# Rotary products of attention moved from VectorE to GpSimd, in a fused attention and two-layer kernel

## The reference, cut to what matters

```python
def _attn_ref(q, k, v):                       # (4, 8, 576, 64) each
    ...
    def rotate(x):
        x1, x2 = (x[..., :half], x[..., half:])
        return np.concatenate([x1 * cos - x2 * sin, x1 * sin + x2 * cos], axis=-1)
    q_rot, k_rot = (rotate(q), rotate(k))
    scores = scale * np.matmul(q_rot, k_rot.transpose(0, 1, 3, 2))
    scores = scores - np.max(scores, axis=-1, keepdims=True)
    attn = np.exp(scores)
    attn = attn / (np.sum(attn, axis=-1, keepdims=True) + 1e-09)
    return np.matmul(attn, v).astype(np.float32)
...
x = attention output as (2304, 512)
h = x @ w_in;  x = (h - np.tanh(h)) @ w_out                     # first layer, d_ff 2048
h = x @ w_in;  x = (h * (1.0 / (1.0 + np.exp(-1.702 * h)))) @ w_out   # second layer
```

## Time and profile before

| what | value |
|---|---|
| median of 3 runs (lowest to highest) | 1146.83 us (1146.66 to 1147.7) |
| the profiled execution's own time | 1147.27 us |
| its span, first to last instruction | 1145.5 us |
| granted clock, mean | 0.997 |
| PE busy | 1104.1 us (96%) |
| DVE busy | 552.4 us (48%) |
| ACT busy | 425.7 us (37%) |
| POOL busy | 57.1 us (5%) |

### The profile page before, as it was taken

How to read it: one execution, slowest core, us unless ns; L and a number is a source line. 1 busy time by engine, 2 the same in 40 slices (tenths; PEclk the granted TensorE clock), 3 DMA queues, 4 the chain that set the end, 5 groups by cost and what they waited for, 6 DMA issues and landing times.

```text
span 1145.5 us, 15078 instructions
## 1 busy us (share of the span) xinstructions
PE 1104.1 (96%) x5952; PEld 1017.8 (89%) x5952; DVE 552.4 (48%) x879; ACT 425.7 (37%) x747; POOL 57.1 (5%) x62
## 2 busy tenths in 40 slices
PE   2999998999999999999999999999999999999998
PEld 1888877787789999999999999999999999999997
DVE  7888887888736433232233333455232322323222
ACT  2555554555544423222222323445232222323222
POOL 3011111102111000000000000000000000000000
PEclk9999999999999999999999999999999999999999
DMA  6355557566315300000000100062000000000000
GB/s 182 95 158 127 155 154 201 136 169 166 87 61 178 102 28 29 28 28 11 19 28 28 29 28 28 1 193 83 28 28 28 28 1 28 28 28 1 28 1 28
DMA packets 78854, 79.85 MB, mean 70 GB/s; under 512 B 30144, under 2 KB 55744, under 8 KB 78784
## 3 DMA queue, kind: packets, MB, share of 16 engines
q1 hardware_dynamic: 78784, 78.89, 24.1%
HBM read 55.12 MB, written 14.23 MB: 61 GB/s over the span
## 4 chain that ended last, share of the span: by engine, by line
PE 89%; DVE 7%; SPq 1%; DMA 1%; POOL 1%; issue 1%; ACT 0%; POOLq 0%; DVEq 0%; ACTq 0%
PE PS L485 35%; PE PS L503 17%; PE PS L500 17%; PE PS L449 10%; PE PS L414 3%; PE PS L431 3%; PE PS L437 3%; DVE neg_max L667 2%; DVE q_max L684 1%; DVE k_hl L679 1%; DVE q_max L674 1%; DMA turned_k<-k_dram 1%; DVE raw_q L662 0%; DVE w_parts L697 0%; DVE raw_q L660 0%
## 5 line engine op out<-in xcount | busy, mean ns | idle before, releaser
L485 PE MATMUL PS<-x_hi,w_parts 128*128 128x384 f32 x1536 | 423.1, 336 | 0.0
L742 DVE TENSOR_TENSOR g_raw<-PS,act_t 128x384 f32<-128x384 f32 x192 | 107.0, 557 | 400.2 <-ACT act_t L610 202.1
L485 PEld LDWEIGHTS PS<-x_hi,w_parts 128*128 128x128 f32 x1536 | 280.5, 188 | 4.3
L485 PE MATMUL PS<-x_lo,w_parts 128*128 128x384 f32 x768 | 257.2, 335 | 0.0
L500 PE MATMUL PS<-g_hi,w_parts 128*128 128x384 f32 x768 | 210.3, 334 | 0.8 <-DVE g_lo L747 0.8
L503 PE MATMUL PS<-w_parts,g_hi 128*128 128x512 f32 x576 | 195.1, 393 | 1.0 <-DVE y_sb L756 0.8
L449 PE MATMUL PS<-probs,v_one 128*128 128x288 f32 x640 | 183.4, 409 | 0.3 <-ACT pv_sb L545 0.3
L747 DVE TENSOR_TENSOR g_lo<-g_raw,g_hi 128x384 fp32r<-128x384 f32 x192 | 107.7, 561 | 113.6 <-ACT g_hi L617 113.6
L537 ACT ACTIVATE probs<-PS 128x576 f32<-128x576 f32 x160 | 104.0, 650 | 129.6 <-PE PS L437 126.3
L485 PEld LDWEIGHTS PS<-x_lo,w_parts 128*128 128x128 f32 x768 | 144.2, 188 | 4.2
L617 ACT ACTIVATE g_hi<-g_raw 128x384 fp32r<-128x384 f32 x192 | 100.8, 525 | 122.9 <-DVE g_raw L742 119.7
(11 more groups left out here) (51 smaller groups left out, 741.3 us busy)
## 6 DMA issues: line engine op xcount, KB each, us to landing
x_raw<-x_scratch SPq DMA_DIRECT2D x12, 768.0 KB, 4.5
raw_w<-moe_w_in_dram SPq DMA_DIRECT2D x32, 256.0 KB, 3.1
raw_w<-moe_w_out_dram SPq DMA_DIRECT2D x32, 256.0 KB, 3.3
raw_k<-k_dram SPq DMA_DIRECT2D x16, 288.0 KB, 3.5
turned_k<-k_dram SPq DMA_DIRECT2D x64, 72.0 KB, 3.2
raw_q<-q_dram SPq DMA_DIRECT2D x16, 288.0 KB, 3.8
turned_q<-q_dram SPq DMA_DIRECT2D x64, 72.0 KB, 3.5
k_one<-k_hl SPq DMA_DIRECT2D x32, 144.0 KB, 2.4
```

Source lines behind the costliest of these rows:

```text
L485: last = nc.tensor.matmul(h_banks[j % 2], w_parts[j][:, w, c * P:(c + 1) * P], x[par][:, c, :], start=(c == 0 and w == 0 and x is x_hi), s ...
L742: nc.vector.tensor_tensor(g_raw[:, j % 2, :], h_banks[j % 2], act_t[:, j % 2, :], ALU.subtract if m == 0 else ALU.mult).then_inc(g_done, 1)
```

## The change

Only the rotary products of pair 0 stay on VectorE (`rope_first`, counted by a new semaphore `first_roped`). Those of pairs 1 to 15 are issued by GpSimd: pair 1 and then pair 2 behind its memsets, and from then on k and q of pair p+2 ahead of `normalise(p-1)`. ScalarE's `keys_hi` and `queries_hi` wait for the counts from GpSimd, except for pair 0. The ones beside the keys are written over 576 columns in place of 640; the last 64 columns keep GpSimd's zeros (they are padding keys, whose rows of v are zero).

```diff
+            def rope(t, pair):
+                par, at = pair % 2, 3 + 4 * (pair - 1) + (2 if t == "k" else 4)
+                pool.wait_ge(loaded[t][par], (pair // 2 + 1) * 80)
+                nc.gpsimd.tensor_tensor(turned[t][par][:, :], turned[t][par][:, :], sin_sb[:, :], ALU.mult).then_inc(pool_chain, 1)
+                nc.gpsimd.tensor_tensor(raw[t][par][:, :], raw[t][par][:, :], cos_sb[:, :], ALU.mult).then_inc(pool_chain, 1)
+                pool.wait_ge(pool_chain, at)
+                nc.gpsimd.tensor_tensor(raw[t][par][:, :], raw[t][par][:, :], turned[t][par][:, :],
+                                        ALU.add).then_inc(k_roped if t == "k" else q_roped, 1)
+
             def normalise(pair):
                 par = pair % 2
+
+                pool.wait_ge(q_roped, min(pair + 3, PAIRS - 1))
                 pool.wait_ge(inv_in[par], pair // 2 * 32 + 32)
...
-            for pair in range(PAIRS - 1):
-                normalise(pair)
+            pool.wait_ge(consts_in, 32)
+            rope("k", 1)
+            rope("q", 1)
+            for pair in range(PAIRS):
+                if pair + 2 < PAIRS:
+                    rope("k", pair + 2)
+                    rope("q", pair + 2)
+                if pair:
+                    normalise(pair - 1)
             normalise(PAIRS - 1)
...
             def keys_hi(h):
-                act.wait_ge(k_roped, h // 2 + 1)
+                if h < 2:
+                    act.wait_ge(first_roped, 1)
+                else:
+                    act.wait_ge(k_roped, h // 2)
...
-            def rope(t, pair):
...
+            def rope_first(t):
+                dve.wait_ge(loaded[t][0], 80)
...
-                last = nc.vector.memset(k_one[j][max_rows(j % 2), :].bitcast(F32), 1.0)
+                last = nc.vector.memset(k_one[j][max_rows(j % 2), 0:SEQ].bitcast(F32), 1.0)
...
             for t in "kq":
-                rope(t, 0)
+                rope_first(t)
             for h in range(-PREPARED, NHEADS):
                 if 0 <= h + 1 < NHEADS:
                     for t in range(1, TILES):
                         row_max(h + 1, t)
-                if 0 <= h and h // 2 + 2 < PAIRS:
-                    rope("kq"[h % 2], h // 2 + 2)
                 if 0 <= h + 1 < NHEADS:
                     place_maxima(h + 1)
-                if -2 <= h < 0:
-                    rope("kq"[h % 2], 1)
```

More of the change, by code:

```diff
@@ L133, in program @@
         q_roped = sem("q_roped")
+        first_roped = sem("first_roped")
         k_hi_done = sem("k_hi_done")
@@ L553, in queries_hi @@
             def queries_hi(h):
-                act.wait_ge(q_roped, h // 2 + 1)
+                if h < 2:
+                    act.wait_ge(first_roped, 2)
+                else:
+                    act.wait_ge(q_roped, h // 2)
                 if h >= 4:
@@ L655, in _ @@
         def _(dve):
-            def rope(t, pair):
-                par, at = pair % 2, pair * 4 + (2 if t == "k" else 4)
-                dve.wait_ge(loaded[t][par], (pair // 2 + 1) * 80)
-                nc.vector.tensor_tensor(turned[t][par][:, :], turned[t][par][:, :], sin_sb[:, :], ALU.mult).then_inc(dve_chain, 1)
-                nc.vector.tensor_tensor(raw[t][par][:, :], raw[t][par][:, :], cos_sb[:, :], ALU.mult).then_inc(dve_chain, 1)
-                dve.wait_ge(dve_chain, at)
-                nc.vector.tensor_tensor(raw[t][par][:, :], raw[t][par][:, :], turned[t][par][:, :],
-                                        ALU.add).then_inc(k_roped if t == "k" else q_roped, 1)
+            def rope_first(t):
+                dve.wait_ge(loaded[t][0], 80)
+                nc.vector.tensor_tensor(turned[t][0][:, :], turned[t][0][:, :], sin_sb[:, :], ALU.mult).then_inc(dve_chain, 1)
+                nc.vector.tensor_tensor(raw[t][0][:, :], raw[t][0][:, :], cos_sb[:, :], ALU.mult).then_inc(dve_chain, 1)
+                dve.wait_ge(dve_chain, 2 if t == "k" else 4)
+                nc.vector.tensor_tensor(raw[t][0][:, :], raw[t][0][:, :], turned[t][0][:, :], ALU.add).then_inc(first_roped, 1)
             def row_max(h, t):
```

## The result

| what | before | changed |
|---|---|---|
| median, both side by side on one chip | 1146.74 us (4 runs) | 1157.37 us (4 runs) |
| ratio, with its interval | | 1.0088 [1.007, 1.0105] |
| profiled execution, span | 1147.27, 1145.5 us | 1157.52, 1155.7 us |

What follows compares the result with a forecast made beforehand. TensorE was taken to bound attention, with ScalarE, not VectorE, releasing `queries_lo`. Terms 4.3 + 4.4 + 0.8 - 1.0 - 0.7 - 1.0 - 1.1 + 3.3 gave +9.0 us, forecast 1155.8 us, range 1149 to 1163.

Steps and rivals of the forecast that it cites:

- the start: Up to the first heads: GpSimd's k products of pairs 1 and 2 hold up VectorE's work, +4.4 us (2 to 5.5).
- the walk: Main case: GpSimd's and VectorE's two-input SBUF products take turns, 1.3 and 0.63 us; +9.0 us in all, chance 0.62.
- The undisturbed turn: Heads 4, 6, 8, 10, 12: GpSimd's products delay `queries_lo` and the `row_max` by 0.85 us each; +4.3 us (1.5 to 8).
- Head 14: TensorE's idle 1.78 us from late `place_maxima` goes, low parts collide for 0.8 instead; -1.0 us.
- head 19: `queries_lo` no longer waits behind the cut of x and `keys_lo`, only for ScalarE; -1.0 us.
- The term of heads 16 to 18: After the weight loads the wait for sums stays, only the collision with `normalise` goes; -0.7 us, head 18 at 0.
- The weight cuts: Heads 21, 23, 25, 27: VectorE's half starts right after ScalarE's, 0.27 us gained in each; -1.1 us.
- The even heads between them: Even heads between the odd heads with cuts collide like the steady ones, 0.83 us each; +3.3 us (1.2 to 6.4).
- Late ropes: Rival: in head 17 GpSimd's products finish late and ScalarE's `queries_hi` waits; 2 to 5 us, 1158 to 1161, chance 0.14.
- Cheap collisions: Rival: `queries_lo` falls into the gap at GpSimd's semaphore wait, 0.3 us or less each; 1150.4 us, chance 0.11.
- Balance: Rival: collisions are cheap and the start costs 2 in place of 4.4; +1.2 us, 1148.0, chance 0.08.
- faster: Rival: VectorE's relief counts and the low parts miss GpSimd's products altogether; 1143.0 us with no collisions, chance 0.05.

Runs made afterwards that it cites:

- number 1: The changed kernel without any rotary product from pair 1 on, on any engine; 1139.15 us, 0.9921 of the kernel before.
- number 2: The changed kernel with memsets of 1440 elements in place of GpSimd's rotary products; 1145.86 us, 0.9979 of the kernel before.
- number 12: The kernel before, plus six idle GpSimd products of 128x576 for each pair, whose results nobody reads; 1209.91 us, 1.0543 of the kernel before.
- number 7: The changed kernel with pairs 1 and 2 on VectorE, GpSimd beginning with pair 3, run a second time; 1157.68 us, 1.0088 of the kernel before.
- the later run: The changed kernel again, unaltered, on another chip; 1155.83 us, 1.0068 of the kernel before.
- number 3: The kernel before with only the ones written over 576 columns in place of 640; 1147.16 us, 0.9996 of the kernel before.
- number 10: The kernel before with only the q products of pairs 11 to 15 on GpSimd, started behind `invert`; 1145.39 us, 0.998 of the kernel before.
- number 8: The changed kernel with pair 1 on VectorE and GpSimd's later products started after the even head's `queries_lo`; 1159.32 us, 1.0093 of the kernel before.
- number 9: The kernel before with only q products of pairs 2 to 15 on GpSimd, after the even head's `queries_lo`; 1150.54 us, 1.0021 of the kernel before.

## Why the prediction was right

**Direction and mechanism: shown. The size: in part luck.** The profile lost 10.3 us where 9.0 was forecast, because the start was put 1.2 too high and all the rest together 2.4 too low. Three experiments carry it from different sides: without the products the heads are at 9.24 again (number 1), with writes in their place both low parts stay at 0.75 (number 2), and with idle reading products alone the heads grow (number 12). The ends in the changed kernel alternate as the walk had them.

**The undisturbed turn, forecast 0.85, measured 1.0 and 0.9 on the mean of two executions.** Two errors nearly cancelled. I charged 0.24 twice for GpSimd's wait on its own semaphore; the rows show 0.08 between the end of one product and the start of the next (94.60 after 94.52, 97.46 after 97.38). Walked with 0.08 the turn costs 0.6 at the place where `normalise` stood before. And I took that place as fixed. It moved by 0.3 to 0.4 on the mean. That is about what the held addition puts ahead of the reciprocal (0.47 in place of 0.17), but the runs do not show that this is the cause. In number 1 the addition took 0.17 and `normalise` still started only 0.13 to 0.44 ahead of the copy in heads 6 to 12; in number 7 it took 0.47 and `normalise` started 1.07 to 1.32 ahead there, nearly as before. Why it moves stays open.

**The start, forecast 4.4, measured 3.24 and 1.80.** The walk to the first `row_max` gave 24.2 against 24.13, but by errors that cancelled: GpSimd began at 11.86 and not 12.6, so all three products of q of pair 0 were held, and the last low part was not. In the later run, with GpSimd from 12.65 on, it was 22.80. M(1,2) went on at 32.20, not 33.2: the loads of pair 2 came in at 27.6, and only `queries_lo` of head 2 was held, `keys_lo` not. So the term hangs on when the k of pair 1 lands: that alone is 1.35 of the 1.44 between the two executions. The matmuls' own variation of up to 1.3 (numbers 3 and 10) comes on top of it.

**The gains.** Head 14 and head 19 came as forecast. The term of heads 16 to 18, -0.7, did not, and it is too small to tell: number 3, which moved no product, had -0.8 there. In the changed kernel +2.56 and -2.58 balance, with a wait of 3.1 us for the sums where the earlier trace rows have 2.78. The weight cuts gave half of -1.1, with 0.25 in three of the four, and head 27 was no gain. The even heads between them cost 3.8 against 3.3, inside their bounds.

**The rivals.** *Late ropes*: the sign named for them, ScalarE waiting for GpSimd at `queries_hi`, came once, 2.4 us for pair 1, with no wait of TensorE behind it (number 8); not seen from pair 2 on; number 8 shows what they would have cost, 1.05 for each odd head. *Cheap collisions*: not seen, the least of the ten steady turns cost 0.59. *Balance* and *faster*: the relief alone is worth 9.1 us, more than the gains that I listed, since it also shortens the start and head 18, and heads 27 and 28 happened to be 1.9 shorter. The contention takes it back twice over.

**The range.** The text says that 1149 to 1163 goes two thirds of the way from the forecast to the lowest and the highest sum. It goes 6.8 of 8.1 and 7.2 of 8.7, over four fifths; by two thirds it would have been 1150.4 to 1161.6, which holds the result too.

## What to carry to other kernels

Before moving a product with two SBUF inputs to GpSimd, list the VectorE instructions with two SBUF inputs that will run beside it, and ask which of them has no slack: each costs up to 1.9 us in place of 0.75, however idle VectorE is on the mean. Place GpSimd's products where VectorE reads only PSUM, and start them by a count of the last instruction that must not be held, small ones included; number 10 did that and gained, number 9 missed one instruction of 0.17 us and lost. A collision at a start that is paced by loads moves to the next load when one pair of work is moved away from it.

## What the runs showed of the hardware that was not expected

- An addition with one SBUF input and 9 elements per partition is held to the end of GpSimd's running instruction: 1.31 us beside a memset, 0.76 beside a product, 0.17 alone. In numbers 8 and 9 and the changed kernel its end is 0.03 behind that of the product each time. A product with two SBUF inputs is not held by a memset (0.75).
- With work ready on both engines neither got two turns in a row in the rows shown: 1.26 to 1.3 for GpSimd, 0.62 for VectorE, and a profile counts the time held as the instruction's own. One row of the later run does not fit: a product of GpSimd from 26.82 on took 2.70, with `place_maxima` and then a `keys_lo` that kept 0.74 inside it.
- TensorE's matmuls reached their short durations later in one execution than in another, with M(1,2) at the same time to 0.01 and the granted clock at 1.00 in both; it moved the first copy by 0.95 us in number 3 and by 1.26 in number 10.
